# Expert rounds: another order of the turns, relu in two evictions, weight units and scaling moved within the round

## What is computed

```python
logits = np.einsum('bsd,de->bse', x, w_gate)
for b in range(B):
    for s in range(S):
        # expert e of the token: its own argmax, or that of the token before it
        p = softmax(logits[b, s])
        h = np.maximum(x[b, s] @ w1[e], 0.0)      # 512 -> 1024
        out[b, s] = p[e] * (h @ w2[e])            # 1024 -> 512
```

## Time and profile before

| | |
|---|---|
| span of the profiled execution | 727.3 us |
| time of that execution | 729.05 us |
| median of three runs | 729.2 us |
| TensorE busy (products) | 714.5 us, 98% |
| VectorE, ScalarE, GpSimd busy | 305.0, 233.8, 130.8 us |
| chain that ended last | TensorE 95% |
| granted TensorE clock | 0.998 |

### The profile page before, as it was taken

The page is one execution under the profiler, slowest core; times in us unless marked ns, Lnnn a source line. Parts: engine busy times, 40 slices in busy tenths (PEclk is TensorE's granted clock), DMA queues, the critical chain, the costliest instruction groups (busy, mean ns, idle before and its releaser), DMA issues.

```text
span 727.3 us, 14145 instructions
## 1 busy us (share of the span) xinstructions
PE 714.5 (98%) x5004; PEld 648.0 (89%) x5005; DVE 305.0 (42%) x641; ACT 233.8 (32%) x451; POOL 130.8 (18%) x166
## 2 busy tenths in 40 slices
PE   7999999999999999999999999999999999999996
PEld 7799999999999999999999999788888788888885
DVE  5765332235332235332224722785445362222441
ACT  2773142023142023142021033321445353121441
POOL 5574020002020002020000016022121212122221
PEclk9999999999999999999999999999999999999999
DMA  9952131012131012100010340114753453111000
GB/s 222 378 107 67 33 99 33 1 35 67 33 99 33 1 35 67 33 33 1 1 38 2 116 163 16 53 44 139 255 179 114 168 194 123 38 43 38 31 24 12
DMA packets 71997, 57.65 MB, mean 79 GB/s; under 512 B 54892, under 2 KB 57228, under 8 KB 71952
## 3 DMA queue, kind: packets, MB, share of 16 engines
q1 hardware_dynamic: 68432, 47.58, 21.9%
q0 software_dynamic: 3520, 9.44, 4.0%
HBM read 48.79 MB, written 10.31 MB: 81 GB/s over the span
## 4 chain that ended last, share of the span: by engine, by line
PE 95%; issue 1%; DVE 1%; ACT 1%; DVEq 0%; POOL 0%; ACTq 0%; POOLq 0%
PE bank L640 42%; PE bank L783 15%; PE bank L808 15%; PE bank L572 5%; PE bank L603 3%; PE bank L795 2%; PE bank L595 2%; PE bank L671 2%; PE bank L725 1%; PE bank L515 1%; PE bank L543 1%; PE bank L560 1%; PE bank L582 1%; PE bank L648 1%; PE bank L529 0%
## 5 line engine op out<-in xcount | busy, mean ns | idle before, releaser
L640 PE MATMUL bank<-u_h,wc_h 128*128 128x288 f32 x384 | 117.2, 305 | 0.1
L640 PE MATMUL bank<-hid_h,wc_h 128*128 128x288 f32 x384 | 115.0, 300 | 0.0
L640 PE MATMUL bank<-hid_l,wc_h 128*128 128x288 f32 x384 | 113.2, 295 | 0.0
L640 PE MATMUL bank<-u_h,wc_l 128*128 128x288 f32 x384 | 113.1, 295 | 0.0
L640 PE MATMUL bank<-u_l,wc_h 128*128 128x288 f32 x384 | 113.1, 294 | 0.0
L640 PE MATMUL bank<-hid_h,wc_l 128*128 128x288 f32 x384 | 113.0, 294 | 0.0
L808 PE MATMUL bank<-wslots,hT_h 128*128 (+1 forms) x336 | 107.8, 402 | 0.5 <-DVE hT_l L1688 0.5
L783 PE MATMUL bank<-wslots,xgT_h 128*128 (+1 forms) x336 | 106.6, 398 | 0.6 <-issue 0.6
L1482 DVE SCALAR_TENSOR_TENSOR hid_l<-bank,hid_h 128x288 fp32r<-128x288 f32 x96 | 43.1, 454 | 108.7 <-ACT hid_h L988 108.2
L988 ACT ACTIVATE hid_h<-bank 128x288 fp32r<-128x288 f32 x96 | 39.2, 409 | 113.6 <-PE bank L640 113.2
L640 PEld LDWEIGHTS bank<-u_h,wc_h 128*128 128x128 f32 x384 | 72.1, 188 | 1.8 <-DVE hid_l L1482 1.0
(11 more groups left out here) (270 smaller groups left out, 1045.6 us busy)
## 6 DMA issues: line engine op xcount, KB each, us to landing
w1raw<-in_moe_w_dram SPq DMA_DIRECT2D x20, 512.0 KB, 3.5
w2raw<-in_moe_w_dram SPq DMA_DIRECT2D x20, 512.0 KB, 5.5
wc_raw<-in_moe_w_ch_dram SPq DMA_DIRECT2D x8, 768.0 KB, 11.2
vb<-in_v_dram SPq DMA_DIRECT2D x32, 128.0 KB, 3.2
x_rows<-x1n SPq DMA_DIRECT2D x16, 256.0 KB, 2.2
kb<-in_k_dram SPq DMA_DIRECT2D x24, 128.0 KB, 3.0
qb<-in_q_dram SPq DMA_DIRECT2D x24, 128.0 KB, 3.0
qraw<-in_q_dram SPq DMA_DIRECT2D x2, 512.0 KB, 4.7
```

The source lines that it names most:

```text
L640: last = pe.matmul(to, lhsT, rhs, start=(m == 0), stop=(m == len(mms) - 1))
```

## The change

- TensorE: the first turn stands behind one group of half 1, before behind two; the turn of the next tile's rows moves behind the first group of the output, directly before the second turn. A turn waits for the first piece of the relu before its first transpose and for the second piece before its third.
- ScalarE: the relu is two instructions of 256 columns. Unit 7 of AFTER_END moves from behind the second hT copy to behind the first; unit 6 from AFTER_END to AT_END; the copy of the next tile's turned rows moves behind the second hT copy.
- VectorE: the loop works for its own tile and scales it at the end; unit 6 of AFTER_END stands behind the first hT_l, xgT_l behind the second. The word `tiles` loses its second element and the instruction that filled it.

```diff
             def hidden(t, n, half, again, chunks):
...
-                    pe.wait_ge(hs_done, 2 * t + half - 1)
+                    pe.wait_ge(hs_done, 2 * (2 * t + half - 1))
...
             def h_turn(t, half, again):
-                pe.wait_ge(hs_done, 2 * t + half + 1)
...
                     f = half * KF // 2 + c
+                    if c % 2 == 0:
+                        pe.wait_ge(hs_done, 2 * (2 * t + half) + c // 2 + 1)
...
                 hidden(t, n, 0, again)
-                hidden(t, n, 1, again, FIRST)
+                hidden(t, n, 1, again, (0,))
                 h_turn(t, 0, again)
-                hidden(t, n, 1, again, SECOND)
+                hidden(t, n, 1, again, (1, 2, 3))
+                output(t, n, 0, again, (0,))
                 x_turn(t + 1)
-                output(t, n, 0, again, (0,))
                 h_turn(t, 1, again)
...
-                act.activation(hs[:, half * 512:(half + 1) * 512], bank[half][:, :], ACT.Relu).then_inc(hs_done, 1)
+                for c in range(2):
+                    act.activation(hs[:, half * 512 + c * 256:half * 512 + (c + 1) * 256], bank[half][:, c * 256:(c + 1) * 256],
+                                   ACT.Relu).then_inc(hs_done, 1)
...
-            units(EARLY, word, AT_END, (4, 5), True)
+            units(EARLY, word, AT_END, (4, 5, 6), True)
...
                 hs_out(t, 0)
-                units(t, word, AFTER_END, (6,), again)
                 hT_out(t, 0)
+                units(t, word, AFTER_END, (7,), again)
                 hs_out(t, 1)
+                hT_out(t, 1)
                 xgT_out(t + 1)
-                hT_out(t, 1)
-                units(t, word, AFTER_END, (7,), again)
...
-                units(t + 1, word, AT_END, (4, 5), again)
+                units(t + 1, word, AT_END, (4, 5, 6), again)
...
-            def tile(before, again):
-                t = before + 1
+            yo_out(EARLY - 1, True)
+
+            def tile(t, again):
                 word = next_weights(t)
-                yo_out(before, again)
+                hT_out(t, 0)
                 units(t, word, AFTER_END, (6,))
-                hT_out(t, 0)
+                hT_out(t, 1)
                 xgT_out(t + 1)
-                hT_out(t, 1)
                 units(t, word, AFTER_END, (7,))
...
                 units(t + 1, word, AT_END, (4, 5))
-
-            last = dve.value_load(tiles[0:1, 1:2], min_val=N // P - 1, max_val=NT - 1)
-            with dve.Fori(EARLY - 1, NT - 1) as before:
-                with dve.If(before < last):
-                    tile(before, again=True)
-
-            yo_out(last, True)
+                yo_out(t, again)
+
+            n = dve.value_load(tiles[0:1, 0:1], min_val=N // P, max_val=NT)
+            with dve.Fori(EARLY, NT) as t:
+                with dve.If(t < n):
+                    tile(t, again=True)
```

More of the change, by code:

```diff
@@ L200, in build @@
             ending = sb(part2, "ending", [1, NTP + 1])
-            tiles = sb(part2, "tiles", [1, 2], I32)
+            tiles = sb(part2, "tiles", [1, 1], I32)
             mx = sb(part2, "mx", [P, J])
@@ L1627, in tables @@
                 beside(dve.tensor_reduce(begun[:, 1:NTP + 1], tg[:, :, :], AX_X, ALU.add))
-                beside(dve.tensor_copy(tiles[:, 0:1], first_tile[0:1, E:E + 1]))
-                then(dve.tensor_scalar(tiles[:, 1:2], first_tile[0:1, E:E + 1], -1.0, None, ALU.add))
+                then(dve.tensor_copy(tiles[:, :], first_tile[0:1, E:E + 1]))
                 beside(dve.tensor_tensor(changed[:, 2:NTP + 2], begun[:, 1:NTP + 1], begun[:, 0:NTP], ALU.not_equal))
```

## The result

The changed kernel took 727.93 us (median of 20 runs, 727.2 to 729.0), the kernel before 729.18 beside it (20 runs). The ratio is 0.9984, with a 95% interval of 0.9977 to 0.9991: 1.25 us faster, where I had forecast 0.6 us slower. The time lies inside the range of 727.2 to 732.0, outside the 728.8 to 730.6 of my own case, and nearest to rival D, 728.4. The profiled execution has a span of 726.5 and a time of 728.29 (before 727.3 and 729.05), at a granted clock of 0.999.

The account below looks back on a forecast made before the run. TensorE's own work was taken to bound the loop, with its only stall in rounds 8 and 9. +2.2 - 0.85 + 0.2 - 0.97 = +0.6 on 729.05 gave 729.65, with 0.15 for the median 729.8 us; range 727.2 to 732.0.

Parts of the forecast that it names:

- my own case: Whole kernel: first turn waits for relu pieces, outweighing the savings; 729.8 us, 728.8 to 730.6, chance 0.42.
- rival D: Expert loop: wait of 0.13 and savings cancel, only the end and round 8 show; 728.4 us, chance 0.12.
- rival A: First turn: it does not wait for the relu, only savings are left; about 726.6 us, chance 0.18.
- The turn's wait: First turn of all 17 rounds: waits for relu pieces and ends 0.13 us late, +2.2 us.
- The savings: Each loop round: 0.03 from hT_l in time, some 0.02 from two turns in a row; together -0.85 us.
- Round 8: Round 8, beyond an ordinary round's terms: +0.5 - 0.5 + 0.2 = +0.2 us.
- w1 late: Round 8's load for w1: units start one copy later in round 7, wait 0.35 becomes 0.85, +0.5 us.
- hT_l late: Round 8: VectorE takes hT_l before unit 6, wait of 0.49 shrinks to 0.1 or so, -0.5 us.
- unit 7 and the gap behind it: End of round 8: waits of 0.36 for unit 7 and 1.06 at the next round's start stay, +0.2 us.
- The end: Program's end: VectorE's last scaling starts 0.22 behind the last product, no longer after 7 empty rounds, -0.97 us.
- B: First turn: both relu waits restart TensorE 0.24 behind ScalarE's end, not 0.05; 0.33 late, 733.2 us, chance 0.15.
- C: First turn: a relu piece takes 0.41, as 288 columns do; 0.20 a round, 731.0 us, chance 0.13.

Follow-up runs that it names:

- the kernel in between: Changed kernel with first turn behind four products, next rows' turn and xgT copies back where they were before: 725.55 us, 0.9957 of the kernel before.
- the relu whole: Changed kernel with the relu as one instruction of 512 columns: 731.55 us, 1.0031 of the kernel before.
- the last experiment: Changed kernel with ScalarE's xgT_h copy back ahead of the second hT_h: 727.74 us, 0.9983 of the kernel before.
- the units undone: Changed kernel with the weight units back at their old places on ScalarE and VectorE: 729.69 us, 1.0007 of the kernel before.
- the units together: Changed kernel with VectorE's unit 7 directly behind unit 6, after the first hT_l: 727.01 us, 0.9972 of the kernel before.
- the turns as before: Changed kernel with TensorE's order and the xgT copies' places as before; two-piece relu, units and scaling kept: 725.94 us, 0.9956 of the kernel before.
- the experiment that has nothing else: Kernel before with only VectorE's loop working for its own tile and scaling it at the round's end: 728.36 us, 0.9985 of the kernel before.

## Why the prediction was wrong, step by step

The forecast is off by 1.85 us (+0.6 for -1.25). Against its terms the ordinary rounds give 0.67 of that (+1.35 forecast, +0.68 measured), round 8 0.73, tile 3 0.29; the rest lies between executions. All three err the same way. That the time still fell inside the range says nothing for the mechanism: the range reached down into rival A.

**The bound** held: the loop is TensorE's own work and the stall is in round 8. So did the sign for an ordinary round.

**The turn's wait** was sized at 0.13 a round and is 0.06 to 0.07. Duration of the piece, overlap and 0.05 from ScalarE's end to the load were all right. The step that failed is "a product begins 0.11 to 0.15 behind a load that is not hidden": in this turn it begins 0.05 to 0.06 behind (load 549.49, product 549.54; from the third load at 549.77 the fourth product follows at 549.94, 0.17 later, of which 0.11 are the third product's step). From load to load around the first turn the cost can be read directly: 549.09 to 549.94 is 0.85 with the wait, 548.64 to 549.43 is 0.79 in the kernel in between, without. Averaged over the 14 rounds, the steps from the turn's first product to the second one behind the turn add up to 0.670 before, 0.671 in the kernel in between and 0.737 after: 0.067. With the relu whole, the round grows by 0.20 more.

**The savings** were sized at 0.05 a round. The 0.03 for hT_l fits: the kernel in between, where nothing waits, has rounds 0.03 under the kernel before, and the steps around the turn of the next rows, averaged in the same way, add up to 0.698 before and 0.671 there. The 0.02 for two turns in a row are next to nothing. A turn alone takes 0.79 from the load before it to the load behind it; 0.23 of that is one ordinary step, and the two loads behind it take 0.34 to the next (549.94 to 550.28) where they otherwise take 0.47, 0.13 given back: 0.43 for the turn. Two in a row take 1.22, less the same 0.36 is 0.86, 0.43 each. So these steps give 0.07 - 0.03 = 0.04 a round, the mean shows 0.042, the forecast had 0.08: 0.6 us too much in 16 rounds.

**Round 8** is where the sign was lost: +0.2 forecast, -0.53 measured. By its terms:

| | forecast | before, after | difference |
|---|---|---|---|
| w1 late | +0.5 | 0.35, 0.20 + 0.61 | +0.46 |
| hT_l late | -0.5 | 0.73, none | -0.73 |
| unit 7 and the gap behind it | +0.2 | 0.36 + 1.06, 0.20 + 1.08 | -0.14 |

The w1 term is right, and the last experiment shows its cause. The other two are mis-sized. hT_l, by 0.23: I priced it at the 0.49 in brackets before the product, but the four loads of the turn ahead of it started at 564.24 and the next load at 565.56, 1.32 later, where it is 0.59 in round 7. What is lost is 0.73. Unit 7 and the gap behind it, by 0.34: I had put a cascade that gets a little worse, and it got a little better. The step that failed is that xgT_l and the branch take "about as long" as VectorE's wait for ScalarE's unit did. Before:

```profile
567.63 0.69 DVE L1688 TENSOR_TENSOR hT_l<-bank,hT_h 128x512 fp32r<-128x512 f32 x1 [1.15 <-ACT hT_h L1104]
568.98 1.23 DVE L1672 TENSOR_TENSOR wslots<-w2raw,wslots 128x1024 f32 x1 [0.66 <-ACT wslots L982]
```

From the start of the second hT_l to that of unit 7 it was 1.35 (568.98 - 567.63) and is 1.21 (568.62 - 567.41), 0.14 sooner, and the load's wait shrank by 0.16. The remaining 0.16 of the 0.73 are 0.04 of w1 and 0.12 of the leads below.

The brackets add to 2.50 before and 2.09 after, the rounds' excess over an ordinary one is 2.08 and 1.51. The wait of 0.22 in the turn, which every round has, is in neither. Each load wait costs some 0.1 to 0.15 less than its bracket: 0.42 over four waits before, 0.58 over four after, 0.76 over five with the units undone (4.11 for 3.35), 0.28 over two with the units together (0.79 for 0.51), 0.24 over two with the turns as before (0.71 for 0.47). I take this for the lead of the loads over the products, so that a wait that is split in two, as w1's, is covered twice. The sums show the 0.1 to 0.15; the split is argued.

**Tile 3** was costed at nothing ("their order hardly changes") and gave 0.29, for a reason that the order does not tell: an instruction less on VectorE.

**The end**: -0.97 forecast, -0.96 measured, and -0.9 in the experiment that has nothing else. VectorE's empty rounds stay hidden behind GpSimd's.

**The rivals.** A is refuted for the wait (there is one in each round, and no ordinary round got shorter) and right in that the first product is on time. B and C are refuted: no restart of 0.24, no piece of 0.41. D came nearest by its number, and not by its mechanism, as the rounds did move; it had the wait and the savings of a round cancel, and they do by less than a half (0.03 of 0.07). That its number fits is luck: it knew neither the gain in round 8 nor that in tile 3.

Of my own tests, "rounds 8 and 9 lose more than 0.5 of their 2.04" is met in substance: against two ordinary rounds of the same kernel they had 2.07 and now have 26.27 - 24.77 = 1.50, 0.57 less.

What the prediction should have asked: is the sooner turn wanted? It shortened a chain that cost 0.03 a round and brought a wait of 0.06, and asked every unit of round 8 sooner. The change without it is the better kernel by 2.0 us.

## What to carry to other kernels

Before a step is pulled forward, compare the price of the wait that it removes with that of the wait it meets; a chain "on the edge" has at most its few hundredths to give. Price a wait on TensorE by its load's bracket less the 0.1 to 0.15 us that each wait was found cheaper here, not by the bracket before the product. And look last at a wait near the end of a loop's round, since it may be paid again at the next round's start: here 0.20 became 1.0.

## What the hardware showed that I had not expected

- A transpose's product began 0.05 to 0.06 us behind a load that had waited, while the pair of 512 columns behind the restart in round 8 took 0.11 more than its 0.62. A load wait of 0.17 in each round, behind products of 512 columns, left rounds of 12.312, where the shortest of all are 12.311.
- In all 13 kernels the excess of round 8 over an ordinary round was the sum of its listed load waits less 0.09 to 0.15 for each wait (without the turn's wait, which every round has).
- A wait of 0.20 of a load six products before the end of a round was followed by 1.08 at the next round's first load; without it none was listed (round 8 12.89 for 13.89). In all eight kernels with a wait at that place, of 0.20 to 0.81, the gap behind it was 1.06 to 1.11, and from the load that had waited to the next round's first load it was 2.28 to 2.33: the size of the wait did not matter. In the kernels with the turns as before and the one in between, 0.54 to 0.55 stood there with no wait near the round's end, so the gap has a second source that the runs do not show.
- One instruction less on VectorE, far ahead in the program, brought the start of hT_l in tile 3 0.35 us nearer to the copy that it waits for (0.13 for 0.48 behind it).
